# Attention and MLP by row blocks: heads inside, blocks of 256 and 320 tokens

## The reference

```python
# q, k, v: (4, 8, 576, 64)
scores = scale * np.matmul(q, k.transpose(0, 1, 3, 2))
kth = np.partition(scores, -32, axis=-1)[..., -32:-31]      # the 32nd largest of a row
scores = np.where(scores >= kth, scores, -1e9)
attn = softmax(scores)
x = np.matmul(attn, v) -> (2304, 512)                       # 4 x 576 tokens, 8 heads x 64

h = x @ w_in                                                # 512 -> 2048
x2 = np.where(h > 0, h, np.exp(np.minimum(h, 0)) - 1) @ w_out   # 2048 -> 512

# top-1 of 8 experts by normalised x2 @ emb; gate = softmax weight of the winner
out[mask] = gate * (np.maximum(x2[mask] @ w1[e], 0) @ w2[e])
```

## Time and profile before

| what | value |
|---|---|
| median of 3 runs | 1377.01 us (1376.68 to 1377.37) |
| the profiled execution's own time | 1376.88 us |
| its span | 1375.1 us |
| mean granted PE clock | 0.933 |
| busy: PE / DVE / ACT / POOL | 1213.9 / 814.6 / 630.2 / 570.2 us |
| DMA | 72.65 MB, 53 GB/s |

### The profile page before, as it was taken

One profiled execution on the slowest core, in us unless ns is written; L12 is line 12 of the kernel. 1 busy time (PEld: TensorE's weight loads), 2 busy tenths in 40 slices (PEclk: granted clock), 3 DMA queues, 4 the chain that ended last, 5 costly groups with the idle time before them and its releaser, 6 DMA issues.

```text
span 1375.1 us, 24331 instructions
## 1 busy us (share of the span) xinstructions
PE 1213.9 (88%) x7809; PEld 937.0 (68%) x7810; DVE 814.6 (59%) x3202; ACT 630.2 (46%) x1483; POOL 570.2 (41%) x758
## 2 busy tenths in 40 slices
PE   4647767899999999999999999999975999999996
PEld 2425444677787787787687778797865677677773
DVE  4987899999888699888789879020325011011110
ACT  3646555775675686676577576331420000000000
POOL 2858886655555565545555645100000111111112
PEclk9867767899999999999999999999986999999998
DMA  3051101010110100100011000000240444425110
GB/s 113 1 179 48 27 14 23 18 27 10 24 26 15 44 10 19 30 25 19 21 25 27 10 19 2 17 1 6 99 176 16 145 170 153 155 74 210 61 32 21
DMA packets 80141, 72.65 MB, mean 53 GB/s; under 512 B 60310, under 2 KB 60310, under 8 KB 79520
## 3 DMA queue, kind: packets, MB, share of 16 engines
q1 hardware_dynamic: 73584, 56.13, 13.0%
q0 software_dynamic: 3760, 10.49, 2.3%
q10 hardware_dynamic: 2688, 4.72, 1.2%
HBM read 61.88 MB, written 11.27 MB: 53 GB/s over the span
## 4 chain that ended last, share of the span: by engine, by line
PE 73%; ACT 2%; issue 2%; DVE 1%; DMA 0%; POOL 0%; DVEq 0%; ACTq 0%; POOLq 0%
PE mlp L587 19%; PE mlp L578 15%; PE sc L692 11%; PE pv_ps L702 10%; PE pv_ps L558 5%; PE sc L526 4%; PE tp L534 3%; PE pv_ps L541 1%; PE mlp L596 1%; PE tp L535 1%; PE tp L672 1%; PE prep_ps L603 1%; PE sc L518 1%; PE prep_ps L499 1%; PE tp L658 1%
## 5 line engine op out<-in xcount | busy, mean ns | idle before, releaser
L430 POOL TENSOR_TENSOR probs<-scores,probs 128x576 f32<-128x576 f32 x144 | 203.3, 1412 | 273.6 <-ACT probs L742 257.5
L587 PE MATMUL mlp<-g,wout 128*128 128x288 f32 x1024 | 270.5, 411 | 0.0
L936 DVE MAX8 top<-larger_of 128x8 f32<-128x288 f32 x576 | 246.7, 450 | 1.5
L587 PEld LDWEIGHTS mlp<-g,wout 128*128 128x128 f32 x1024 | 187.7, 191 | 61.2 <-issue 17.3
L945 DVE MATCH_REPLACE8 larger_of<-top,larger_of 128x288 f32<-128x288 f32 x432 | 189.6, 445 | 0.0
L578 PE MATMUL mlp<-x_h,win_h 128*128 128x288 f32 x512 | 163.5, 319 | 0.4 <-DVE g L1053 0.2
L692 PEld LDWEIGHTS sc<-xg_t,w_exp 128*128 128x128 f32 x1344 | 155.0, 194 | 11.3 <-issue 11.3
L526 PE MATMUL sc<-k_t,q_t 64*128 64x288 f32 x512 | 127.6, 527 | 35.0 <-ACT k_t L724 20.5
L692 PE MATMUL sc<-xg_t,w_exp 128*128 x1344 | 155.2, 277 | 1.4 <-ACT act_tick L876 1.4
L578 PE MATMUL mlp<-x_l,win_h 128*128 128x288 f32 x512 | 151.5, 296 | 0.0
L578 PE MATMUL mlp<-x_h,win_l 128*128 128x288 f32 x512 | 151.4, 296 | 0.0
(11 more groups left out here) (165 smaller groups left out, 1687.4 us busy)
## 6 DMA issues: line engine op xcount, KB each, us to landing
w_exp<-in_moe_w SPq DMA_DIRECT2D x16, 2048.0 KB, 11.3
x_rows<-g ACTq DMA_DIRECT2D x24, 192.0 KB, 2.1
raw_qk<-in_q SPq DMA_DIRECT2D x32, 128.0 KB, 2.4
raw_qk<-in_k SPq DMA_DIRECT2D x32, 128.0 KB, 2.4
vals<-in_v SPq DMA_DIRECT2D x32, 128.0 KB, 2.4
g<-in_moe_w_in SPq DMA_DIRECT2D x4, 1024.0 KB, 5.5
wout<-in_moe_w_out SPq DMA_DIRECT2D x1, 4096.0 KB, 17.3
raw_qk<-in_q SPq DMA_DIRECT2D x32, 16.0 KB, 2.3
```

The costliest lines, as they stand in the source:

```text
L430: pool.tensor_tensor(pr, scores[:, T % NSC, :], pr, ALU.subtract).then_inc(mask_done, 1)
L587: mm = pe.matmul(mlp_ps[bank_][:, 0:HS], wout[:, c, i * P:(i + 1) * P], g[:, c * HS:(c + 1) * HS], start=(c == 0), stop=(c == FC - 1))
L936: ins = dve.max(ranks(T, half, 8 * r, 8 * r + 8), folds(T, half))
```

## The change

Each pair's rows are taken in two *units*: rows 0-255 (two groups, four tiles) and rows 256-575 (two groups and the mixed tile, five tiles). The units of a batch go in the order rows 0-255 of pairs 0 to 3, then rows 256-575 of pairs 0 to 3. q is loaded and prepared for each unit, k for the first unit of a pair only and kept (`k_t` and `vals` hold four pairs). The MLP's blocks are these same rows, 256 and 320 tokens, each with its own `x_h` and `x_l`, so that a batch's list of positions starts after the first units: batch 0's at slot 24 in place of 44. Block 0's down steps are cut in six parts, block 1's in four: 75 positions; the last three, rows steps, are done in the first slot of the next batch's list. The rows steps take five tiles a batch (128, 128, 128, 96, 96 tokens) in place of six of 96. `x_h` and `x_l` are made per unit, in the slot five after its last tile (`whole_in`). The high half of `w_in` moves from POOL to ACT, and 32 pieces are split over slots 1 to 21. `w_out` (4 MB) is loaded before the q and k of unit 2.

```diff
-        def mlp_slot(s):
-            b, m = divmod(s - LAG - TB, TB)
-            return (b, m) if 0 <= b < B - 1 else None
+        START = NPAIR * TPU[0] + LAG
+
+        def mlp_steps(s, pos):
+            b, m = divmod(s - START, TB)
+            if not 0 <= b < B or s >= END:
+                return []
+            left = [(b - 1, m_, pos_) for m_ in range(TB, MLP_STEPS) for pos_ in range(2)]
+            return (left if pos == 0 and m == 0 and b else []) + [(b, m, pos)]
...
+        def whole_in(s):
+            T = s - XT
+            if 0 <= T < NT:
+                u, t = place(T, TPU)
+                if t == TPU[unit(u)[1]] - 1:
+                    return u
+            return None
...
+            PARTS = (6, 4)
...
+        def pieces_in(s):
+            return [divmod(n, 8) for n in range(8 * KD) if 1 + n * 2 // 3 == s]
+
+        LEFT = END - START - TB * (B - 1)
...
+            def load_raw(u):
+
+                b, blk, j = unit(u)
+                wait(sp, prep_done, ahead(u, PPU))
+                for hh in range(2):
+                    head = q[b, 2 * j + hh, :, :]
+                    sp.dma_start(raw_q[:, 0:2, hh, :],
+                                 head[2 * P * blk:2 * P * (blk + 1), :].rearrange("(c p) d -> p c d", p=P)).then_inc(raw_in, 16)
+                    if blk:
+                        sp.dma_start(raw_q[0:TAIL, 2, hh, :], head[FULL * P:S, :]).then_inc(raw_in, 16)
+                    else:
+                        head = k[b, 2 * j + hh, :, :]
...
-            load_pair(1)
-            load_vals(1)
-            load_w_in(2)
+            load_raw(1)
+            load_vals(0, 1)
             sp.dma_start(wout[:, :, :], w_out.rearrange("(c p) n -> p c n", p=P)).then_inc(wout_in, 16)
-            load_pair(2)
-            load_vals(2)
-            load_w_in(3)
-            for p in range(3, NP):
-                load_pair(p)
-                load_vals(p)
+            for u in range(2, NU):
+                load_raw(u)
+                b, blk, j = unit(u)
+                if blk == 0:
+                    load_vals(b, j)
+                if u in (3, 4):
+                    load_w_in(u - 1)
...
@@ PE and ACT, in the loop over slots
-                if t in (5, 6) and p + 1 < NP:
-                    prep(p + 1, t - 5)
+                if nxt == 0 and t in (0, 1):
+                    prep(u + 1, t)
+                if nxt == 1 and t in (1, 3):
+                    prep(u + 1, t // 2)
...
-            for m in range(MLP_STEPS):
+            for m in range(LEFT, MLP_STEPS):
                 mlp(B - 1, m, 0)
                 mlp(B - 1, m, 1)
...
@@ ACT
-                xp, xt = divmod(s - PT_ - XT, PT_)
-                if xt == 0 and xp >= 0:
-                    x_high(xp)
+                if whole_in(s) is not None:
+                    x_high(whole_in(s))
```

More of the change, by code:

```diff
@@ L29, in attention_moe_program @@
     NCH = FULL + 1
[L30 to L36, removed]
+    NB = (2 * P, S - 2 * P)
+    GPU = (2, 3)
+    TPU = (4, 5)
+    SPU = (8, 10)
+    PPU = (3, 2)
+    RPU = (6, 4)
+    TB = NPAIR * sum(TPU)
+    NU = 2 * NPAIR * B
+    NT = TB * B
     NSC = FULL + 2
@@ L86, in attention_moe_program @@
         wout = sbuf(first, "wout", [P, FC, DM])
[L87 to L92, removed]
+        g = sbuf(first, "g", [P, FC * NB[1]])
+        x_h = [sbuf(first, f"x_h{i}", [P, NPAIR * NB[i]], F32R) for i in range(2)]
+        x_l = [sbuf(first, f"x_l{i}", [P, NPAIR * NB[i]], F32R) for i in range(2)]
+        raw_q = sbuf(first, "raw_q", [P, 3, 2, D])
+        raw_k = sbuf(first, "raw_k", [P, NCH, 2, D])
+        q_t = sbuf(first, "q_t", [P, 2, 2 * P])
+        k_t = sbuf(first, "k_t", [P, NPAIR, S])
         q_diag = sbuf(first, "q_diag", [P, P])
-        vals = sbuf(first, "vals", [P, 2, NCH, 2 * D])
+        vals = sbuf(first, "vals", [P, NPAIR, NCH, 2 * D])
         scores = sbuf(first, "scores", [P, NSC, S])
@@ L188, in head_of, with whole, mixed @@
+        def group_of(T):
+            u, t = place(T, TPU)
+            return ahead(u, GPU) + t // 2
+        def whole(G):
+            return place(G, GPU)[1] < 2
+        def mixed(T):
+            return place(T, TPU)[1] == 4
         def head_of(T):
[L189 to L193, removed]
+            t = place(T, TPU)[1]
+            return t % 2 if t < 4 else 0
         def starts_group(T):
-            return T % PT_ % 2 == 0
+            return place(T, TPU)[1] % 2 == 0
@@ L242, in mlp_schedule @@
                 for d in range(KD):
-                    parts = 5 if KD * blk + d < SPARE else 4
-                    positions += [[("down", blk, d, part, parts)] for part in range(parts)]
-            positions += [[("rows", 1, i, 0, 1)] for i in range(RB)]
+                    positions += [[("down", blk, d, part, PARTS[blk])] for part in range(PARTS[blk])]
+            positions += [[("rows", 1, i, 0, 1)] for i in range(len(ROWS[1]))]
             used, by_act, chunk, numbered = [0, 0], [0, 0], [0, 0], []
@@ L288, in _ @@
         def _(sp):
[L289 to L296, removed]
+            def load_raw(u):
[9 more added lines that the diff above has]
+                        head = k[b, 2 * j + hh, :, :]
+                        sp.dma_start(raw_k[:, 0:FULL, hh, :],
@@ L489, in _, with prep @@
             made = {"prep": 0, "logits": 0}
-            def prep(p, r):
+            def prep(u, r):
+                b, blk, j = unit(u)
                 if r == 0:
-                    wait(pe, raw_in, 128 * (p + 1))
+                    wait(pe, raw_in, 16 * (ahead(u, RPU) + RPU[blk]))
                 wait(pe, prep_evac, made["prep"])
                 wait(pe, logits_out, made["logits"])
-                if r < 2:
-                    for c in range(FULL):
-                        last = pe.transpose(prep_ps[:, c * P:(c + 1) * P],
-                                            raw_qk[:, r, c, :, :].rearrange("p a d -> p (a d)"), ident[:, :])
-                else:
-                    for i in range(2):
-                        last = pe.transpose(prep_ps[:, i * P:(i + 1) * P],
-                                            raw_qk[:, i, FULL, :, :].rearrange("p a d -> p (a d)"), ident[:, :])
+                if r == 0:
+                    parts = [raw_q[:, c, :, :] for c in range(2)]
+                elif blk:
+                    parts = [raw_q[:, 2, :, :]]
+                elif r == 1:
+                    parts = [raw_k[:, c, :, :] for c in range(FULL)]
+                else:
+                    parts = [raw_k[:, FULL, :, :]]
+                for c, part in enumerate(parts):
+                    last = pe.transpose(prep_ps[:, c * P:(c + 1) * P], part.rearrange("p a d -> p (a d)"), ident[:, :])
                 last.then_inc(prep_done, 1)
@@ L821, in _ @@
             for s in range(END):
-                p, t = divmod(s, PT_)
-                if t in (5, 6) and p + 1 < NP:
-                    prep(p + 1, t - 5)
+                u, t = place(s, TPU)
+                nxt = unit(u + 1)[1] if u + 1 < NU else None
+                if nxt == 0 and t in (0, 1):
+                    prep(u + 1, t)
+                if nxt == 1 and t in (1, 3):
+                    prep(u + 1, t // 2)
                 G = scored_in(s)
```

321 lines of the change are left out of this document (177 added, 144 removed).

## The result

The changed kernel takes 1333.82 us (median of 4 runs, 1331.87 to 1334.76) against 1377.19 us (median of 4): a ratio of 0.9682, 95% interval 0.9665 to 0.9698. It is 3.2% faster. The forecast was 1350.9 us, faster, in a range of 1322 to 1372. The range holds the time, and the gain is 43 us where 26 were forecast. Of the bands of the forecast it falls in that of the first rival (1322 to 1337), not in the forecast's own (1337 to 1357).

The account below looks back on a forecast made before the run. DVE bounds the attention stage, leaving PE idle time before the MLP to be won. 146 + 3 x 224.4 + 104.5 + 425.4 = 1349.1 us of span, plus 1.8, gives 1350.9 us; range 1322 to 1372.

Parts of the forecast that it names:

- the first rival: At the copies of x: ACT's slack hides the new wait everywhere, 20 us less, 1330.9 us; chance 0.20.
- Part A: From the start to the first MLP matmul, moved from slot 44 to slot 24: 146 us.
- the new wait: ACT's copy of x, one slot earlier, waits for DVE's normalisation: 3.4 us before the MLP, 4.5 a batch, 3 at the end.
- w_out's place: Before the MLP: w_out's load ahead of unit 2's q and k makes PE wait in slot 4, 4 us.
- Part B: One batch's 36 slots of MLP beside attention, three times: 224.4 us each, from 218.2 before.
- 2 for mixed tiles: In each batch period: two of the four mixed tiles now meet DVE-bound slots, +2 us.
- The three left-over row tiles: In the slot that opens the next batch's list: three of a batch's five row tiles, 2.4 us each.
- Part C: The last 20 slots, first block of batch 3, in which attention runs out: 104.5 us.
- Part D: The rest, from the last batch's second block to the end: 425.4 us, from 423.3 before.
- The second: At the start: load order brings unit 2's q and k late by 13 us, w_in's pieces behind; 1363 us; chance 0.12.
- The third: At the 32 copies of x: the wait is on the path, 2.5 us a copy, slower, 1411 us; chance 0.10.
- The fourth: In block 0's light down slots: PE's clock falls, +1.7 us in 40 slots, slower, 1419 us; chance 0.03.

Follow-up runs that it names:

- the halves later: The first follow-up experiment: high and low halves of x made six slots after a unit's last tile instead of five, against the changed kernel; 1306.39 us.
- the five parts: Block 0's down steps cut in 5 parts instead of 6, against the changed kernel; 1313.92 us.
- the three together: Changed kernel with halves of x one slot later, block 0's down steps in 5 parts, and w_out's load behind unit 2's q and k; 1293.91 us.
- w_in's high half on POOL: w_in's high half moved back from ACT to POOL in the same slots, against the kernel with the halves later; 1314.51 us.
- slots 24, 25, 26 and 28: The three together with the MLP's list starting at each of these slots: 1293.91, 1303.16, 1288.72 and 1292.95 us.

## Why the prediction was right, and where it was not

**What bounds the kernel, and where the gain comes from: right.** The attention stage has PE to spare, and moving the MLP's start from slot 44 to 24 puts 20 slots of it there. The time fell, and 8 slots later cost 2.1 us a slot before the period's own change.

**Part A: right in its sum (146 against 145.7), from terms that were off both ways.** The first threshold came at 28.15, not 30.15. The 22 slots after it lasted to 143.60, 115.5 us, where the sum has 114.7, and the first matmul comes 2.1 behind that threshold, not 1.1: -2.0 + 0.8 + 1.0 = -0.2. Inside the 22 slots, by the thresholds, the new wait cost 4.3 (111.1 with the halves later) where 3.4 were put down, and w_out's place 1.6 where the sum has 4. The rest, 115.5 - 5.9 = 109.6, is 2.3 dearer than the 107.3 written; the preparations, put at 0.7 a slot, may be the place, but no run took them away.

**The added wait: right in its mechanism, too small in its size.** The step of the prediction was "3.4 + 3 x 4.5 + 3 less", 20 us; measured 27.4. In the profiled executions it is 4.5 in A, 7.3 a period and 1.5 in C, less 2.3 in D, which is no finding (below). ACT stood 35 us over 32 copies, 1.1 each, less than the 50 to 90 I looked for. The 3.7 us of standing that the sum reads from the earlier trace rows did not come: there ACT had dropped its tile long before DVE's threshold, and in the change it is as late as DVE itself, having stood for PE's scores before:

```profile
104.05 0.70 ACT L797 COPY scores<-sc 128x288 f32<-128x288 f32 x2 [3.67 <-PE sc L580]
...
105.55 0.79 ACT L804 ACTIVATE probs<-scores,thr 128x576 f32<-128x576 f32 x1
106.84 0.41 ACT L837 CAST x_h<-x_f 128x256 fp32r<-128x256 f32 x1 [0.49 <-DVE x_f L1064]
```

The stages of a period show which copies were under-priced (us a period; the cost is the change less the halves later):

| two copies each in | forecast | ACT stood | cost |
|---|---|---|---|
| block 0's hidden slots | 3.0 | 3.9 | 2.6 |
| block 0's down slots | 0.3 | 2.0 | 1.0 |
| block 1's hidden slots | 1.0 | 1.7 | 3.8 |
| block 1's down slots | 0.3 | 0.4 | 0.0 |

In block 0's hidden slots the mechanism and the price are as forecast: one threshold interval changed by 6.72 - 5.49 = 1.2 us where the sum has 1.5. In block 1's, where PE was to hide part of it, it did the opposite: PE stood 2.3 to 2.6 us ahead of the row tile, and the clock fell behind it. Where it was low for 6.8 us the stage is 5.1 us longer than with the halves later, where it was low for 3.4 us 3.2 longer. So the cost is not a share of what ACT stood: it depends on who stands behind ACT. With the five parts in place the wait was worth less: from the five parts to the three together it is 20.0 (the runs of the five parts scatter over 10), and 3.2 of that is w_out's.

**Part B: 224.4 against 223.5, again by errors that cancel.** Without the wait the period is 216.2, and the sum has 224.4 - 4.5 = 219.9. By stages the sum has, without the wait, 45.0, 59.5, 51.7 and 61.8, and 2 for mixed tiles; the kernel with the halves later shows 44.2, 59.6, 51.5 and 60.9. So the two larger cuts (the down steps in six parts, the wider matmuls of block 1) were priced well, and the 2 us for mixed tiles don't show. (Slips of arithmetic are small: 6.4 x 0.485 + 2.19 is 5.29 and not 5.33, which would make the sum 0.4 higher; 12.2/2 is 6.10 and not 6.07.) The three left-over row tiles, 2.4 each in the sum, take 8.3 us, 2.8 each, and behind them the hidden steps start slow: block 0's hidden stage is 44.9 and 44.2 us in the batches that have them ahead, 43.3 in the one that hasn't. Freeing them by the five parts took 7.7 a period with the wait in place and 1.8 without. One term of the sum agrees with the trace: the down products of block 1 last 34.47/64 = 539 ns (485 + 54). Two rows of the chain of waits, the last batch's MLP (start, length, engine, line, count):

```profile
921.53 20.10 PE mlp L633 x132
941.64 34.47 PE mlp L642 x128
```

**Part C is the step that failed: 104.5 against 89.8, 15 of the 19 us by which the span was missed.** It has "three left-over row tiles 7.2" in it. They are run ahead of the first hidden step, and so are inside the third period, where B had counted them already. The other 7.5 are spread over the part. From its first hidden matmul to its first down product it is 46.5 us (816.3 to 862.8), and 43.3 from there. The sum, if both mixed tiles and both waits are put down to the hidden slots, has 50.2 and 47.1: 3.7 and 3.8 too much. The second is the slots in which attention runs out, for which the sum takes no row of the kernel before, though its last slots before 892.4 are such; the first has 4 us for mixed tiles, which did not show in B either.

**Part D: right** (425.4 against 424.0; among the runs it moves from 423.9 to 426.3 with nothing changed in it, so 1.4 is no finding).

**The rivals.** The first, that ACT's slack hides the wait, gave 1330.9 and lies nearest to 1333.8, yet it is the one that the first experiment refutes: the wait is on the path for 27 us. The sum is too high by 15 us in C, which happens to bring the time near the rival's. That it fell there is luck, and so is it that B came out near. The second, a start spoilt by the load order, is wrong: a wait of 7 us on PE was there, and 2 to 3 reached the end. The third needed 1.44 us a copy to turn the sign; it was 27.4/32 = 0.86. The fourth, the clock: the light slots held it but for 3.4 us in batch 0. A window over block 0's down slots of that batch, in which PE is 56.2 of 58.7 us busy:

```profile
191.40:250.10 58.70, 56.17 (x375) 42.57 (x373) 55.43 (x234) 38.28 (x90) 38.76 (x50) 0.97 0.17 39
```

The whole stage takes 61.4 us there and 60.1 in the two batches in which the clock held, 5.1 and 5.0 a slot; the sum has 4.74. With w_in's high half on POOL it fell for 3.4 us in these slots in every batch. But the transposes didn't hold the clock down there, as the rival had it, from the section "Part 4: PE-mode transpose" of the Trainium skill's "TensorE: Matmul & The Clock Gate". It did fall elsewhere: among the row tiles and behind PE's 2.3 to 2.6 us of standing in block 1. That activity releases the clock, as the section "What's actually happening" of the same page of the Trainium skill has it, agrees with the 0.72 of the leftover slot, where PE stood between row tiles. But with the three together it fell at 557.2, where PE had been busy 4.16 of 5.20 us, mostly with transposes and row tiles, and it stayed low over 10.2 us of unbroken work. Whether the standing or the kind of work decides among the row tiles, the runs don't part.

## What to carry to other kernels

When a step is moved in a loop that all engines share, ask of which slot its input comes, on each engine, and not only whether the buffer is free: one slot here was worth 27 of the 71 us that the kernel with the halves later wins. Ask also who stands behind the engine that waits: the same copy cost nothing in one stage and about 2 us in another. A time that agrees with a rival's number is no evidence for its mechanism; only taking the wait away told the two apart. Sum a schedule by cutting it at instructions that both traces have, and count a piece that crosses a cut in one part only.

## What the runs showed that was not expected

- The period depends on where the MLP's list begins against the score tiles, and not smoothly: 214.4, 216.8, 211.5 and 212.9 us for slots 24, 25, 26 and 28.
- PE's clock is part of it. With the list from slot 26 all three periods have a granted clock of 1.00, with the change 0.96 to 0.97. In each of the change's three periods it falls in two places: where the copy of x holds PE up ahead of a row tile, and at the three row tiles one behind another.
- A hidden matmul starts 120 ns after the one before it at 256 columns, 132 or 133 at 288 (the kernel before) and 147 at 320 (medians at the upper level), 213 at 256 columns at the lower level: some 13 ns for 32 columns, as the sum had it.
- Taking 13 us of work off POOL and giving ACT 10 for it was worth 8 us, though neither is the busiest engine of that stretch: 4.2 us of it came in that stretch and 1.9 in each period.
